# Transposing a chunk's output for the router: from TensorE to block moves on chip and VectorE

## The reference

```python
x = attention(q, k, v)                               # (2304, 512)
xn = x / sqrt(mean(x * x, axis=-1) + 1e-6) * rms_g   # the MLP
g = xn @ w_gate                                      # 512 -> 1536
y = (g * sigmoid(g) * (xn @ w_val)) @ w_out          # 1536 -> 512
logits = y @ moe2_w_gate                             # the router, 512 -> 8
noisy = logits + log1p(exp(y @ moe2_w_noise)) * noise
top2 = the two largest of noisy, weights = softmax over the two
out = sum over the two of weight * (relu(y @ w1[e]) @ w2[e])
```

## Time and profile before

| | us |
|---|---|
| median of 3 runs | 1107.4 (1107.07 to 1108.57) |
| the profiled execution | 1106.87 |
| its span in the trace | 1105.0 |
| TensorE busy | 1076.4 (97%) |
| VectorE busy | 575.4 (52%) |
| ScalarE busy | 324.3 (29%) |
| GpSimd busy | 398.7 (36%) |
| DMA queue of SP, share of the 16 DMA engines | 22.9% |

### The profile page before, as it was taken

One profiled execution on the slowest core, in us unless ns is written; L12 is line 12 of the kernel. 1 busy time (PEld: TensorE's weight loads), 2 busy tenths in 40 slices (PEclk: granted clock), 3 DMA queues, 4 the chain that ended last, 5 costly groups with the idle time before them and its releaser, 6 DMA issues.

```text
span 1105.0 us, 20155 instructions
## 1 busy us (share of the span) xinstructions
PE 1076.4 (97%) x6113; PEld 939.6 (85%) x6114; DVE 575.4 (52%) x1209; ACT 324.3 (29%) x713; POOL 398.7 (36%) x370
## 2 busy tenths in 40 slices
PE   8999999999999999999999999999999999999994
PEld 7878999999998999999987788888888888888883
DVE  6776335254353353353447765565565565565461
ACT  7996123232331432432352102030303020200341
POOL 3557993022022022020185306070706051431485
PEclk9999999999999999999999999999999999999998
DMA  7975527013013012010084526271625253422675
GB/s 215 274 242 192 172 86 276 1 58 115 1 58 116 1 62 92 1 58 1 28 249 159 139 61 186 43 204 38 196 51 170 65 148 92 117 73 61 171 229 187
DMA packets 167356, 129.40 MB, mean 117 GB/s; under 512 B 96720, under 2 KB 128864, under 8 KB 167296
## 3 DMA queue, kind: packets, MB, share of 16 engines
q1 hardware_dynamic: 145440, 71.20, 22.9%
q10 hardware_dynamic: 16032, 38.47, 10.5%
q0 software_dynamic: 5824, 18.95, 5.1%
HBM read 85.87 MB, written 42.73 MB: 116 GB/s over the span
## 4 chain that ended last, share of the span: by engine, by line
PE 87%; POOL 3%; issue 3%; DMA 2%; ACT 2%; DVE 1%; another core or an unknown queue 0%; SPq 0%; POOLq 0%; ACTq 0%; DVEq 0%
PE bank L793 26%; PE bank L957 19%; PE bank L973 18%; PE bank L825 13%; PE bank L986 3%; PE bank L739 2%; PE bank L766 1%; POOL token_rows_a L680 1%; PE bank L749 1%; PE bank L733 1%; DMA token_rows_b<-expert_rows,slots_u 1%; PE bank L861 1%; ACT p_sb L1108 1%; POOL token_rows_a L693 1%; PE bank L872 1%
## 5 line engine op out<-in xcount | busy, mean ns | idle before, releaser
L793 PE MATMUL bank<-x_parts,mlp_weights 128*128 128x384 f32 x1704 | 312.0, 337 | 0.4 <-issue 0.3
L793 PEld LDWEIGHTS bank<-x_parts,mlp_weights 128*128 128x128 f32 x1704 | 296.8, 188 | 6.3 <-issue 1.2
L957 PE MATMUL bank<-expert_parts,xT_high 128*128 (+1 forms) x688 | 216.6, 396 | 1.5 <-DVE xT_low L1653 1.5
L973 PE MATMUL bank<-expert_parts,hT_high 128*128 (+1 forms) x688 | 213.3, 391 | 3.9 <-DVE hT_low L1664 3.9
L662 POOL TENSOR_TENSOR expert_parts<-raw_expert_a,expert_parts 128x512 fp32r<-128x512 f32 x64 | 81.4, 1304 | 240.6 <-ACT expert_parts L1255 240.4
L825 PE MATMUL bank<-mlp_weights,hidden_parts 128*128 128x512 f32 x648 | 162.2, 394 | 1.3 <-ACT y_sb L1179 1.3
L973 PEld LDWEIGHTS bank<-expert_parts,hT_high 128*128 128x128 f32 x688 | 129.7, 189 | 31.7 <-POOL expert_parts L662 2.8
L957 PEld LDWEIGHTS bank<-expert_parts,xT_high 128*128 128x128 f32 x688 | 125.6, 188 | 26.1 <-issue 2.2
L825 PEld LDWEIGHTS bank<-mlp_weights,hidden_parts 128*128 128x128 f32 x648 | 120.0, 188 | 25.1 <-ACT y_sb L1179 1.6
L973 PE MATMUL bank<-expert_parts,hT_low 128*128 (+1 forms) x344 | 134.6, 391 | 0.0
L957 PE MATMUL bank<-expert_parts,xT_low 128*128 (+1 forms) x344 | 134.3, 390 | 0.0
(11 more groups left out here) (206 smaller groups left out, 1225.1 us busy)
## 6 DMA issues: line engine op xcount, KB each, us to landing
raw_expert_a<-in_w ACTq DMA_DIRECT2D x32, 512.0 KB
raw_expert_b<-in_w ACTq DMA_DIRECT2D x32, 512.0 KB, 4.5
x_row<-routed_rows SPq DMA_DIRECT2D x172, 64.0 KB
expert_rows<-y_row SPq DMA_DIRECT2D x43, 256.0 KB
expert_rows<-zeros SPq DMA_DIRECT2D x4, 2304.0 KB, 12.6
v_sb<-in_v SPq DMA_DIRECT2D x32, 256.0 KB, 3.5
q_sb<-in_qT SPq DMA_DIRECT2D x16, 288.0 KB, 3.7
k_sb<-in_kT SPq DMA_DIRECT2D x16, 288.0 KB, 4.1
```

What stands on the lines that cost most here:

```text
L793: last = nc.tensor.matmul(bank[:, 0:CHUNK], w_sb[:, i, wp, at:at + P], xp[:, par, part, k, :], start=n == 0, stop=n == 3 * KB - 1)
L957: last = nc.tensor.matmul(ps[half][:, 0:512], (xTh, xTl)[xp][:, buf, k, :], ew_sb[:, bass.ds(slot, 1), wp, k * F2 + half * 512:k * F2 + ha ...
L973: last = nc.tensor.matmul(ps[5][:, 0:D], (hTh, hTl)[hp][:, f, :], ew_sb[:, bass.ds(slot, 1), 2 + wp, f * D:(f + 1) * D].rearrange("p a n - ...
```

## The change

For chunks 0 to 4 the transposes leave TensorE. Once `y_ready` has the three tiles of chunk c, SP issues 16 transfers from `y_sb` to a new buffer `y_blocks` (the memory of `xc`): source quarter q of the partitions, column blocks s, to destination quarter s, block q, each 32 partitions by 12 runs of 32 numbers (128 bytes, 48 KB in all). After step 3's gate DVE waits for all 16 and transposes three tiles within their 32 by 32 blocks into `yT_sb`. In `pe_logitsT` TensorE waits for that as before.

`y_blocks` and `xc` share their memory, so SP's order becomes: wait for `xl_ready`, wait for `y_ready`, 16 block transfers, wait for `yT_copied`, then the load of the next x and the zeros. The next x is so issued after step 3 of the chunk, not after step 10 of the one before. Only chunk 1's x is loaded as before. The last chunk keeps its transposes on TensorE.

```diff
@@ -160,6 +160,8 @@
+    y_blocks = at("y_blocks", [P, CHUNK_TILES, D], F32, mlp.pos)
     under = Area(mlp.pos)
@@ -288,6 +290,7 @@
         y_ready = sem("y_ready")
+        y_blocks_in = sem("y_blocks_in")
         yT_done = sem("yT_done")
@@ -448,6 +451,16 @@
+        def load_y_blocks(sp, c):
+            sp.wait_ge(y_ready, CHUNK_TILES * (c + 1))
+            for q in range(BLOCKS):
+                for s in range(BLOCKS):
+                    sp.dma_start(
+                        y_blocks[s * BLOCK:(s + 1) * BLOCK].rearrange("r t (k q c) -> r t k q c", k=KB, c=BLOCK)[:, :, :, q],
+                        y_sb[q * BLOCK:(q + 1) * BLOCK].rearrange("r t (k s c) -> r t k s c", k=KB, c=BLOCK)[:, :, :, s]
+                        ).then_inc(y_blocks_in, 16)
         def load_block(sp, i, thirds=(0, 1, 2)):
@@ -493,6 +506,9 @@
                 sp.wait_ge(xl_ready, KB * c)
+                if c >= 2:
+                    load_y_blocks(sp, c - 2)
+                    sp.wait_ge(yT_copied, ONE + CHUNK_TILES * (c - 1))
                 load_chunk(sp, c)
@@ -506,6 +522,9 @@
+            sp.wait_ge(xl_ready, KB * CHUNKS)
+            load_y_blocks(sp, CHUNKS - 2)
@@ -836,11 +855,11 @@
-        def yT_places(c, t):
+        def yT_of(c, t):
             if isinstance(c, int) and c == CHUNKS - 1:
-                return ps[3 + t], yT_last[:, t]
-            return BANK_A, yT_sb[:, t]
+                return yT_last[:, t]
+            return yT_sb[:, t]
@@ -848,17 +867,11 @@
-        def pe_yT(pe, c, t):
-            n = CHUNK_TILES * c + t
-            bank, _ = yT_places(c, t)
-            pe.wait_ge(y_ready, n + 1)
-            if bank is BANK_A and t == 0:
-                pe.wait_ge(rms_ready, CHUNKS if isinstance(c, int) and c >= CHUNKS - 2 else c + 2)
-            if bank is BANK_A and not (isinstance(c, int) and n == 0):
-                pe.wait_ge(yT_copied, ONE + n)
+        def pe_yT(pe, t):
+            pe.wait_ge(y_ready, CHUNK_TILES * (CHUNKS - 1) + t + 1)
             for k in range(KB):
-                last = nc.tensor.transpose(bank[:, k * P:(k + 1) * P], y_sb[:, t, k * P:(k + 1) * P], ident[:])
+                last = nc.tensor.transpose(ps[3 + t][:, k * P:(k + 1) * P], y_sb[:, t, k * P:(k + 1) * P], ident[:])
             last.then_inc(yT_done, 1)
@@ -867,10 +880,13 @@
             pe.wait_ge(yT_copied, ONE + CHUNK_TILES * (c + 1))
+            if not (isinstance(c, int) and c == CHUNKS - 1):
+                pe.wait_ge(rms_ready, c + 2)
             for k in range(KB):
                     last = nc.tensor.matmul(lgT_bank(c)[LOGITS * t:LOGITS * (t + 1), 0:P], rw_sb[:, k, :],
-                                            yT_places(c, t)[1][:, k, :], start=k == 0, stop=k == KB - 1,
+                                            yT_of(c, t)[:, k, :], start=k == 0, stop=k == KB - 1,
                                             skip_group_check=True)
@@ -917,8 +933,6 @@
                 if not first:
-                    if 1 <= i <= 3:
-                        pe_yT(pe, c - 1, i - 1)
                     if i == 4:
@@ -993,7 +1007,7 @@
             for t in range(CHUNK_TILES):
-                pe_yT(pe, c, t)
+                pe_yT(pe, t)
             pe_up2(pe, 0, 0, 0, 0, (1,), {2: lambda: pe_logitsT(pe, c), 3: lambda: pe_logits(pe, c)})
@@ -1416,14 +1430,17 @@
-        def dve_yT(dve, c, t):
-            n = CHUNK_TILES * c + t
-            dve.wait_ge(yT_done, n + 1)
-            bank, to = yT_places(c, t)
-            if bank is BANK_A and not (isinstance(c, int) and n == 0):
+        def dve_yT(dve, c):
+            dve.wait_ge(y_blocks_in, 16 * BLOCKS * BLOCKS * (c + 1))
+            if not (isinstance(c, int) and c == 0):
                 dve.wait_ge(lgT_done, ONE + c)
-            nc.vector.tensor_copy(to.rearrange("p k t -> p (k t)"), bank[:]).then_inc(yT_copied, 1)
+            for t in range(CHUNK_TILES):
+                nc.vector.transpose(yT_sb[:, t].rearrange("p k t -> p (k t)"), y_blocks[:, t, :]).then_inc(yT_copied, 1)
+        def dve_yT_last(dve, t):
+            dve.wait_ge(yT_done, t + 1)
+            nc.vector.tensor_copy(yT_last[:, t].rearrange("p k t -> p (k t)"), ps[3 + t][:]).then_inc(yT_copied, 1)
@@ -1497,8 +1514,8 @@
                 if not first:
-                    if 1 <= i <= 3:
-                        dve_yT(dve, c - 1, i - 1)
+                    if i == 3:
+                        dve_yT(dve, c - 1)
                     if i == 4:
@@ -1686,7 +1703,7 @@
             for t in range(CHUNK_TILES):
-                dve_yT(dve, c, t)
+                dve_yT_last(dve, t)
             dve_logitsT(dve, c)
```

## The result

The changed kernel takes 1096.96 us in the median (1096.55 to 1098.5, 5 runs), against 1107.4 us (1105.79 to 1108.57, 5 runs). The ratio is 0.9911, with a 95% interval of 0.9897 to 0.9925.

What follows compares the result with a forecast made beforehand. The prediction took TensorE to bound the kernel, with 87% of the chain. Transposes removed, 6.5 us, plus the stall at the branch, 1.45 us, made 7.9 us: 1107.4 - 7.9 = 1099.5 us, range 1098.0 to 1103.5.

Steps and rivals of the forecast that it cites:

- What bounds the kernel: In the MLP an instruction taken off TensorE is worth its time there; TensorE holds 87% of the chain.
- The transposes removed: TensorE, steps 1 to 3 of five chunks: 15 groups of four transposes at 0.43 us each, 6.5 us gained.
- The block transfers: SP's 16 transfers per chunk: landed 12.3 us after y, within 19.1 us of room, at no cost on the path.
- The far bounds: Block transfers at worst: 84 ns per packet read from SBUF, 32 us for the chunk.
- The series of 40 us: Rival: the 16 block transfers go one after the other, 21 us late five times, about 1204 us; chance 0.02.
- VectorE: Its three transposes per chunk, 2.15 us after step 3's gate, find the blocks there and delay nothing; cost nothing.
- SP and the moved x: Next x issued at about 203.8 us; squares on POOL end 12 us or more before TensorE needs them; cost nothing.
- The second gain: Step 0 of chunk 3, at the loop's branch: with x and zeros moved away, its excess of 1.45 us goes.
- only the transposes: Rival: the stall at the branch stays as long, or moves; only 6.5 us gained, 1100.9 us; chance 0.32.
- a fetch's latency alone makes the stall: At the loop's branch: the stall is all latency, so the gain there is 0 and the time 1100.9 us.
- The sum: Whole kernel: 6.5 + 1.45 = 7.9 us gained, 1099.5 us, with the expert stage moving as a whole.
- The first rival: Blocks come late, TensorE waits before the router's matmuls in step 4 of each chunk: 1130 or 1180 us; chance 0.09.

Runs made afterwards that it cites:

- 48 transfers: The changed kernel with each block transfer cut in three, one per tile, 48 of 16 KB per chunk: 1174.04 us, ratio 1.0603.
- third trace of the changed kernel: The changed kernel run a third time with no edit, on the same chip as the next two runs: 1097.46 us.

## Why the prediction was right or wrong

- **What bounds the kernel** was right. TensorE's steps set the MLP's time, and the instructions removed there were worth what they took.
- **The transposes removed**, 15 x 0.43 = 6.5 us: right. All 15 steps are 0.43 shorter, and putting the transposes back returns them.
- **The block transfers** were right in kind and size. I took 12.3 us to the landing; it was about 12.2. That it fits so well is luck: 16 issues took 10.69 us where I had 16 x 0.582 = 9.3, and the landing behind them 1.4 us where I had 3. The issue took 0.62 us in the median where the loads of the earlier trace rows had 0.58. The far bounds are off the table: 6400 packets at 37.2% of 16 engines in 13 us (184.6 to 197.6) are 12 ns each, also with SBUF as the source. The series of 40 us did not come either: each transfer took 2.0 us to land, and they overlapped.
- **VectorE** was right. No wait, 1.89 us for three transposes from SBUF to SBUF where I had 2.15 from the row with PSUM as target.
- **SP and the moved x** were right. x was issued at 203.24 (I had 203.8), the squares ran from 208.75 to 215.56 (by my terms, 203.8 + 5.5 or 11.2 + 7.0, their end is 216 to 222 and not the 217 to 223 that I wrote), and TensorE never waited for their sum. One VectorE instruction was stretched to 1.27 us beside them, without effect.
- **The second gain**, at the branch: the mechanism was right for step 0 of chunk 3, whose 1.45 us came back in full. The term was too small, since I took that step of the earlier trace rows alone. The step ahead of it lost 0.6 us, to TensorE's own code fetches, which the prediction doesn't have: half of it stays when the traffic is moved, and all of it goes with the transposes. Together it was 2.05 us in that trace. x and zeros late, and nothing else, shorten the MLP by 1.7 us in the traces; the means of all executions differ by 2.1 +- 0.4 us, 1.4 in one comparison and 3.1 in the other. The case "only the transposes", to which I had given 0.32, is refuted, and so is the reading that a fetch's latency alone makes the stall. That "the programs' lengths shift", which I had counted for that case, happened, and made a gain.
- **The sum.** 6.5 + 2.05 would have been 8.55 us and 1098.9. That lies inside my range, and the measured gain of 10.4 does not. What failed is the step "the expert stage is expected to move as a whole", and with it that everything outside the MLP was put at nothing. Of the 10.4 us between the medians the MLP has 8.3; 1.1 lie in the rest and 0.5 in the start. The last 0.5 is there because the profiled execution of the kernel before lay 0.5 below its median, and that of the changed kernel did not. The sum lets none of these three change. Two traces of the kernel before differ by 1.7 us in the rest, and the range had 0.9 us for all spread below my best case. Single executions of the kernel before reach from 1104.6 to 1112.0. The changed kernel's mean is 10.0, 10.8 and 11.3 us shorter in the three comparisons: 8.4 in the MLP, and 1.6 to 2.9 behind or around it. Whether the change causes those, the runs don't settle.
- **The first rival** did not come, but its price was too low. At 48 transfers the lateness cost 16.2 us in chunk 1 for a wait of 13.7, since the clock fell. Whether a lateness of 1 to 2 us, where the change would begin to lose, costs the clock too is not shown: a wait of 1.28 us did not, one of 2.57 did.

## What to carry to other kernels

A transpose that is not urgent can leave TensorE for block moves on chip and VectorE's transposes within blocks, and is then worth its difference in step time, provided that issue time by transfer (0.6 to 0.67 us each here) times their number stays inside the slack. Count a bulk transfer not only against the data that waits for it but also against the place where the program branches back. Look at the code fetches of each engine in a loop's second pass: here a program shorter by 24 transposes no longer needed TensorE's. Leave room in a range for every stage that begins with waits for other engines or for DRAM, also if the change doesn't touch it, and take that room from several executions rather than one.

## What the runs showed of the hardware

- A transfer of 128-byte runs from SBUF to SBUF costs SP 0.60 to 0.62 us in the median to issue, with 384 runs or with 128, and lands 2.0 or 1.8 us after its issue. Its packets take 12 ns each on a DMA engine.
- At a branch back over a long loop body, VectorE stood still for 5.24 and 4.20 us while 2.3 MB of zeros were in flight; with the DMA engines idle (share 0.02 and 0.00) it had only its waits for ACT and TensorE. By the Trainium skill (Runtime: NRT & Kernel Launch, Instruction fetch mechanics) such a branch forces a fetch of the target by DMA; the runs add that the stall's length comes from the traffic it meets.
- TensorE's code was fetched 9 times from 310 to 480 us in the kernels with the transposes, and not once in the changed kernel.
- With a wait of TensorE of 2.57 us came 3.4 us at a granted clock of 0.50, and with one of 13.7 us 13.7 us of it, which reached 5.3 us beyond the wait. A wait of 1.28 us brought none, nor did waits of 1.23 and 1.44 us 8 us apart in the third trace of the changed kernel.
